# Another order for ScalarE's softmax steps and TensorE's max-out groups in a fused attention and expert kernel

## The reference

```python
scores = scale * np.matmul(q, k.transpose(0, 1, 3, 2))         # 4 x 8 heads, 576 x 576, head_dim 64
kth = np.partition(scores, -top_k, axis=-1)[..., -top_k:-top_k + 1]   # top_k = 32
scores = np.where(scores >= kth, scores, -1000000000.0)
attn = np.exp(scores - np.max(scores, axis=-1, keepdims=True))
attn = attn / (np.sum(attn, axis=-1, keepdims=True) + 1e-09)
x = np.matmul(attn, v)                                         # then laid out as 2304 x 512
...
h = np.maximum(np.maximum(x @ w1, x @ w2), x @ w3)             # 512 -> 768, three ways
x = h @ w_out                                                  # 768 -> 512
...
logits = x @ w_gate + modality_bias[modality_id]               # 8 experts
e_idx = np.argmax(logits, axis=1)                              # gate_w is its softmax value
for e in range(E):
    mask = e_idx == e
    h = np.maximum(x[mask] @ w1[e], 0.0)                       # 512 -> 1024
    out[mask] = gate_w[mask, None] * (h @ w2[e])
```

## Time and profile before

| | us |
|---|---|
| median of 3 runs | 944.2 |
| the three runs | 942.74, 952.32, 944.2 |
| the profiled execution, its own time | 942.74 |
| its span in the trace | 941.1 |
| PE busy in the span | 894.8 (95%) |
| DVE busy | 719.8 (76%) |
| POOL busy | 660.9 (70%) |
| ACT busy | 568.1 (60%) |

### The profile page before, as it was taken

How to read it: one execution, slowest core, us unless ns; L and a number is a source line. 1 busy time by engine, 2 the same in 40 slices (tenths; PEclk the granted TensorE clock), 3 DMA queues, 4 the chain that set the end, 5 groups by cost and what they waited for, 6 DMA issues and landing times.

```text
span 941.1 us, 17738 instructions
## 1 busy us (share of the span) xinstructions
PE 894.8 (95%) x5132; PEld 690.0 (73%) x5133; DVE 719.8 (76%) x2191; ACT 568.1 (60%) x1274; POOL 660.9 (70%) x624
## 2 busy tenths in 40 slices
PE   5588999999999999999999999999999999999997
PEld 2244868668685777759686786858685898998996
DVE  6999999999999999999999999999803721251211
ACT  3577778678777787778786787766614322341221
POOL 7999998988988799878988889885462421231221
PEclk8699999999999999999999999999999999999999
DMA  7621212321211212122221221111052161116110
GB/s 253 210 59 47 60 44 71 96 84 44 71 47 56 69 48 70 44 71 59 58 57 46 82 60 55 47 37 37 23 164 79 40 228 41 53 32 236 45 56 33
DMA packets 69271, 70.84 MB, mean 75 GB/s; under 512 B 15456, under 2 KB 50560, under 8 KB 69184
## 3 DMA queue, kind: packets, MB, share of 16 engines
q1 hardware_dynamic: 65264, 59.44, 20.9%
q0 software_dynamic: 3920, 10.40, 3.5%
HBM read 59.05 MB, written 10.76 MB: 74 GB/s over the span
## 4 chain that ended last, share of the span: by engine, by line
PE 80%; issue 6%; DVE 5%; ACT 3%; POOL 3%; another core or an unknown queue 1%; DMA 0%; SPq 0%; DVEq 0%; POOLq 0%; ACTq 0%
PE m_ps L1426 18%; PE m_ps L1508 11%; PE m_ps L1452 9%; PE o_ps L1399 8%; PE s_ps L1491 8%; PE t_ps L1383 6%; PE m_ps L1440 6%; PE s_ps L1366 4%; PE o_ps L1491 3%; PE s_ps L1361 2%; DVE top L1154 2%; PE t_ps L1361 2%; PE m_ps L1459 2%; PE m_ps L1445 1%
## 5 line engine op out<-in xcount | busy, mean ns | idle before, releaser
L811 POOL TENSOR_TENSOR scores<-scores,below 128x576 f32<-128x576 f32 x144 | 201.5, 1420 | 63.2 <-ACT below L944 62.7
L1426 PE MATMUL m_ps<-xT,w_sb 128*128 128x192 f32 x1152 | 200.3, 328 | 2.0 <-POOL w_sb L833 2.0
L1426 PEld LDWEIGHTS m_ps<-xT,w_sb 128*128 128x128 f32 x1152 | 185.6, 190 | 5.8 <-issue 5.7
L1154 DVE MAX8 top<-upper 128x8 f32<-128x288 f32 x384 | 159.3, 448 | 0.3 <-issue 0.3
L979 ACT COPY probsT<-t_ps 128x384 f32<-128x384 f32 x240 | 106.7, 492 | 37.7 <-PE t_ps L1383 37.6
L1156 DVE MATCH_REPLACE8 upper<-top,upper 128x288 f32<-128x288 f32 x288 | 125.4, 443 | 0.2 <-issue 0.2
L952 ACT ACTIVATE probs<-scores,shift 128x576 f32<-128x576 f32 x144 | 111.7, 782 | 17.4 <-issue 12.0
L1383 PEld LDWEIGHTS t_ps<-ident,probs 128*128 128x128 f32 x720 | 86.0, 141 | 44.6 <-issue 19.5
L819 POOL TENSOR_SCALAR probs<-probs,inverse 128x576 f32<-128x576 f32 x144 | 106.1, 762 | 16.4 <-DVE inverse L1144 16.4
L1383 PE MATMUL t_ps<-ident,probs 128*128 128x128 f32 x720 | 103.4, 274 | 12.8 <-ACT probsT L979 12.8
L944 ACT ACTIVATE below<-scores,steep_kth 128x576 f32<-128x576 f32 x144 | 109.4, 777 | 2.2
(11 more groups left out here) (208 smaller groups left out, 1777.5 us busy)
## 6 DMA issues: line engine op xcount, KB each, us to landing
k_sb<-keys_t SPq DMA_DIRECT2D x48, 288.0 KB, 2.7
v_sb<-values SPq DMA_DIRECT2D x48, 256.0 KB, 2.7
raw<-e_w SPq DMA_DIRECT2D x12, 1024.0 KB
maxout_rows<-x_rows SPq DMA_DIRECT2D x18, 256.0 KB, 2.2
q_sb<-queries_t SPq DMA_DIRECT2D x48, 64.0 KB, 2.5
w_sb<-w SPq DMA_DIRECT2D x2, 1536.0 KB, 8.4
q_rest<-queries_t SPq DMA_DIRECT2D x96, 16.0 KB, 2.3
v_sb<-values SPq DMA_DIRECT2D x48, 32.0 KB, 2.7
```

The lines of the kernel that those rows point to most:

```text
L811: nc.gpsimd.tensor_tensor(scores[:, r % RING, i, :], scores[:, r % RING, i, :], below[:, i, :], ALU.subtract).then_inc(masked_ready, 1)
L1154: nc.vector.max(best, src).then_inc(topk_step, 1)
L1426: ins = nc.tensor.matmul(dst[:, a * BLK:(a + 1) * BLK], w_sb[:, w, c, (first + a) * P:(first + a + 1) * P], xT[:, m % 2, c, b % SPAN * BLK ...
```

## The change

Five things are edited. `scalars` and `under0` get the number 9 in place of 8, so that `rectify` (8) now comes before them. The group T1 of the superblock before moves from the head of part 0 to the end of part 1; A(2,1), which had been the last group of part 1 with number 10, so becomes one with number 9, and ACT copies it before the steps with number 9. In the last superblock Y0 moves from behind H1 to in front of H0, and Y1 stands before Y2. The special number 5 of the groups W falls away: they have 3 now, so ACT copies W, H0 and H1 before exp1 and exp2.

```diff
-THIS_ROUND = {"scalars": 8, "under0": 8, "under1": 9}
+THIS_ROUND = {"scalars": 9, "under0": 9, "under1": 9}
...
-PARTS = [(late(TURN[1]) + own(A[0]), own(A[1]), own(A[2])),
-         (own(A[3]), own(A[4]), own(A[5])),
+PARTS = [(own(A[0]), own(A[1]), own(A[2])),
+         (own(A[3]), own(A[4]), own(A[5]) + late(TURN[1])),
...
-    ([], own(Y[0]), [])] + PARTS[3:6] + [
-    (own(Y[2], Y[1]), own(X[1], X[2]), []),
+    (own(Y[0]), [], [])] + PARTS[3:6] + [
+    (own(Y[1], Y[2]), own(X[1], X[2]), []),
...
-        elif items[n][2][0] == "W":
-            at.append(5)
```

## The result

| | us |
|---|---|
| before, median of 13 runs (942.48 to 952.33) | 944.59 |
| changed, median of 13 runs (953.24 to 957.84) | 955.32 |
| ratio, 95% interval | 1.0082 [1.0061, 1.0103] |
| changed, profiled execution: time, span | 951.53, 949.9 |
| PE, DVE, POOL, ACT busy in the span | 901.1, 719.2, 660.9, 567.1 |

The change makes the kernel slower by 0.6 to 1.0%. The ratio compares the runs as a whole (the means are 947.5 and 955.6 us). The medians alone would give 1.0114, because the 13 runs before fall into two groups, seven at 942.48 to 944.59 and six at 950.84 to 952.33 us, and their median is the top of the lower group.

What follows compares the result with a forecast made beforehand. POOL bounds the start until the first A, then PE, almost without gaps. Terms 0.6 + 0 + 2.1 + 1.6 + 3.4 = +7.7 us on 942.7 give 950.4; forecast 951, between that and 951.9, range 944 to 956.

Steps and rivals of the forecast that it cites:

- forecast's own case: Whole kernel: the forecast's terms hold and the time falls at 949.5 to 953 us; chance 0.48.
- W groups, +0.6: Rounds 2 to 5: exp2 ends about 1.1 us later, DVE runs late, ACT's copies shift in the first superblock; +0.6 us.
- `rectify` first, 0: Parts 1, 2, 5 and 6: under0 comes later, but POOL's third subtraction waits for under2 anyway; 0 us.
- T1 and the numbers, +2.1: Superblocks 1 to 4, part 2: ACT copies H0 late, PE gaps 0.5 us before H2, four times; +2.1 us.
- Y0, +1.6: Round 48: with Y0 in front of H0, ACT copies H2 later and V starts later; +1.6 us, bounds 1.0 to 2.0.
- Y1 before Y2, +3.4: Round 52: if ACT's idle recurs, PE waits 3.8 us for `rectify` between Y1's parts; +3.4 us, otherwise -0.3.
- waiting for instructions behind big transfers: Around 702 to 709 us: ACT's 6.59 us idle read as waiting for its instructions while the expert's weights load.
- The low clock behind a gap: Rival: round 52's new 3.8 us gap lowers PE's clock, costing 2.1 to 4 us more, 953 to 955 us; chance 0.15.
- The kernel was not faster anywhere: Rival: time not higher, earlier ACT copies in part 3 remove five 1.2 us gaps; 940 us, chance 0.05.
- the gaps at H2: Rival: PE's gaps before H2 in part 2 don't arise and the rest holds; 949 us, chance 0.1.
- PE's waits for probsT: Sign, 135 to 640 us: their sum goes from 5.7 to about 8 us, with four new 0.5 us gaps before H2.
- `full_sum`: Sign, start of the kernel: DVE's first wait at this step grows from 0.7 to about 1.8 us.

Runs made afterwards that it cites:

- change_again: The changed kernel unaltered, run again for a second trace; median 954.61 us, 1.0043 of before [1.0025, 1.0061].
- w_only: The kernel before with only the W edit (ACT copies W, H0 and H1 before exp1 and exp2); 1.0005 of before [0.9996, 1.0015].
- numbers_again: The kernel before with only `scalars` and `under0` at 9, run again for a trace; 951.1 us, where before had a median of 949.41.
- t1_and_numbers: The kernel before with only T1 at the end of part 1 and `scalars` and `under0` at 9; 1.0057 of before [1.0043, 1.0071].
- before_again: The kernel before, unaltered, run again for a second trace; 948.87 us, where before had a median of 949.41.
- y12_only: The kernel before with only Y1 ahead of Y2 in round 52; 0.9999 of before [0.9987, 1.0011].
- hold_load: The kernel before, with the first expert's four 1 MB weight loads held until ACT has copied the last A group; 1.0008 of before [0.9987, 1.0029].
- numbers_only: The kernel before with only `scalars` and `under0` at 9; 1.001 of before [0.9996, 1.0025], its profiled execution, 4719 us, not used.

## Why the prediction held and where it didn't

The sum, +7.7 us, came out near the traced +8.8, and 951 us lay 0.5 under the traced execution. The median, 955.32, lies 4.3 above the forecast, outside the forecast's own case (949.5 to 953) and 0.7 inside the end of the range; it is above the 953.6 that I had called over 1% slower, while the ratio, 0.82%, is under it. That the sum fits the trace is luck in part: W's term was 2.8 us too small and T1's 1.15, and the 3.4 of Y1 before Y2, which the trace doesn't have, made up for most of that. T1's and Y0's mechanisms were right.

- **W groups, +0.6.** From the eighth to the ninth V the traced execution lost 3.4 us (wait 1.49, low clock 1.66; 0.43 of it comes without any lag of DVE, as change_again shows), and w_only's median is +0.4. The step that failed is "exp2 ends about 1.1 us later": with the clock full it ends as before, with the clock low in front of the W group 1.5 us and more later. "Who feels that is ACT in the first superblock" was right, but I had not followed ACT's stream from `kth` on to the copy of V that A(3,0) needs.
- **`rectify` first, 0.** Right by itself (numbers_again: 0.0), though it decided where W's lag came out.
- **T1 and the numbers, +2.1.** Mechanism and places right, size 3.25 (t1_and_numbers: 3.24). ACT's copy of H0 was forecast for 452.66 us; it started at 458.09, which is 452.64 less the shift of 5.45. What I missed lies on PE's side: H2 itself started 0.60 us late, not 0.5, and took 0.11 us more, which I put down to its second half waiting for H1's copy. That makes 0.71 of each step; why the fourth is 0.97 stays open.
- **Y0, +1.6.** Measured 1.71 five times out of five.
- **Y1 before Y2, +3.4.** No trace shows it: there is no idle in the traced execution, and where there is one, before's order (before_again, 262.0 us from the last V on) lost as much as the new (y12_only, 262.7). The step that failed is the reading that Y2 and Y1 cover the idle. They did so in one of the five traces that have both the idle and before's order, by where it fell. The reading "waiting for instructions behind big transfers" failed as well, by hold_load, as far as the 1 MB loads go. The prediction held the idle against the rule in the Trainium skill ("Runtime: NRT & Kernel Launch", section "Instruction fetch mechanics"). What ACT waits for is open, so no run here shows whether the two disagree. The -0.3 us for the swap that I worked out by it was nearer than my 3.4 to what y12_only measured (0.9999 [0.9987, 1.0011]).
- **Rivals.** The low clock behind a gap is real: all seven traces with a gap of 2.3 to 4.5 us in rounds 51 and 52 have it there, and none of the six without (three of these have one later, at 727 to 734 us). It just isn't the swap's, since before's order has the gap too. The kernel was not faster anywhere; the gaps at H2 did arise.
- **The signs.** PE's waits for probsT 7.7 (said 8), V of round 48 1.71 later, first A at 95.96 (said 95.8): right. `full_sum` 2.10 (said 1.8) is off. No wait in round 52 (said 3.8) is wrong for this execution; the second trace has 4.34.

What stays open: the changed kernel cost 0.82% in one comparison and 0.43% in another, where the fixed terms (3.25 + 1.7) are 0.52%; the rest is W's lag and the places of the low clock and of ACT's idle, which differ from one execution to the next, and no run separates them.

## What to carry to other kernels

Two edits that each fit into an engine's slack can together cost what neither costs alone. Here 1.7 and 0.5 us ahead of one copy cost 0.0 and 0.1 us a superblock, and both together 0.8. So add up everything that is put ahead of one copy before calling it hidden. Follow a late result through the stream of the engine that waits for it until you reach every copy that PE needs, not only the next one. And when one execution shows a gap that no edit explains, look at a second trace of the same kernel before pricing an edit by it.

## What the runs showed of the hardware

- PE's granted clock falls to 0.50 at places that change between executions of one kernel: the first A group, behind its 2.0 us wait, took 4.52 us in five traces and 2.84 in four. The changed kernel's first trace has it at 150 to 154 us and its second at 678 to 681, beside other places.
- ACT stands idle 4 to 8 us around 700 to 714 us in all seven traces of two chips and in none of the four of a third, and before's median there is 950.7 and 949.4 us against 943.1. Of the first pair of traces, whose chip isn't known, before's has the idle and the changed kernel's hasn't.
- One execution of numbers_only took 4719 us: PE was busy 4702.1 us with the same 5132 matmuls, ACT 610.6 us, hardly more than its 568.1, and the trace holds no record of a lowered clock. One of before's 27 runs on the same chip took 1308.04 us, at a mean granted clock of 0.654.
